# Moving the normalising operations out of block 0's groups, and a new order at the doors of a three-block gated layer

## What is computed

```python
# 4 batches, 8 heads, 576 positions, 64 wide
ret = (q @ k.T / 8) * Dmat            # Dmat: gamma ** (i - j) below the diagonal
x = (ret @ v)                         # as rows: 2304 tokens x 512
rms = np.sqrt(np.mean(x * x, axis=-1, keepdims=True) + 1e-06)
xn = x / rms * rms_g
g = xn @ w_gate                       # 512 -> 1536
val = xn @ w_val
x = silu(g) * val @ w_out             # 1536 -> 512, silu(g) = g * sigmoid(g)
...                                   # then the routed layer
```

## Time and profile before

| | us |
|---|---|
| median of 3 timed runs | 882.36 (881.67 to 883.47) |
| the profiled execution | 893.08 |
| its span | 891.1 |
| busy in the span: PE, DVE, POOL, ACT | 803.2, 519.7, 450.9, 425.7 |
| granted PE clock, mean | 0.964 |

### The profile page before, as it was taken

One profiled execution on the slowest core, in us unless ns is written; L12 is line 12 of the kernel. 1 busy time (PEld: TensorE's weight loads), 2 busy tenths in 40 slices (PEclk: granted clock), 3 DMA queues, 4 the chain that ended last, 5 costly groups with the idle time before them and its releaser, 6 DMA issues.

```text
span 891.1 us, 14837 instructions
## 1 busy us (share of the span) xinstructions
PE 803.2 (90%) x5053; PEld 706.5 (79%) x5053; DVE 519.7 (58%) x798; ACT 425.7 (48%) x815; POOL 450.9 (51%) x384
## 2 busy tenths in 40 slices
PE   7997688877899999789999999972999999999995
PEld 6886578776679999667999978842888888888884
DVE  3577678998535888653688632351455454554553
ACT  3564464444445555354655423521355454455453
POOL 3568976667754888664688523156112112222221
PEclk9998899999999999799999999987999999999998
DMA  9982012113121223212124012311545545556553
GB/s 317 318 285 86 24 49 70 48 48 95 48 60 36 72 88 125 76 55 60 29 76 143 28 47 67 123 37 32 172 144 163 185 155 169 177 160 173 161 169 103
DMA packets 48362, 99.65 MB, mean 112 GB/s; under 512 B 7490, under 2 KB 8644, under 8 KB 48295
## 3 DMA queue, kind: packets, MB, share of 16 engines
q1 hardware_dynamic: 42934, 87.40, 31.1%
q0 software_dynamic: 4944, 10.96, 4.2%
q10 hardware_dynamic: 432, 0.63, 0.2%
HBM read 89.50 MB, written 10.40 MB: 112 GB/s over the span
## 4 chain that ended last, share of the span: by engine, by line
PE 70%; POOL 10%; DVE 9%; issue 5%; ACT 3%; another core or an unknown queue 2%; DMA 1%; SPq 0%; POOLq 0%; ACTq 0%; DVEq 0%
PE banks L1392 7%; PE banks L1394 6%; PE banks L1393 6%; PE banks L1446 5%; PE banks L1579 5%; PE banks L1580 5%; PE banks L1448 5%; PE banks L1447 5%; PE banks L1581 5%; PE banks L1379 4%; PE banks L1380 4%; PE banks L1381 4%; POOL AL L493 3%; POOL AL L487 2%
## 5 line engine op out<-in xcount | busy, mean ns | idle before, releaser
L1392 PE MATMUL banks<-BH,AH 128*128 128x384 f32 x504 | 175.4, 348 | 29.7 <-DVE g L779 13.3
L1393 PE MATMUL banks<-BL,AH 128*128 128x384 f32 x504 | 171.2, 340 | 0.0
L1394 PE MATMUL banks<-BH,AL 128*128 128x384 f32 x504 | 171.1, 339 | 0.0
L1392 PEld LDWEIGHTS banks<-BH,AH 128*128 128x128 f32 x504 | 96.0, 191 | 41.5 <-DVE g L779 16.5
L809 DVE TENSOR_TENSOR hidL<-hid,hidH 128x384 fp32r<-128x384 f32 x72 | 55.8, 780 | 91.9 <-ACT hidH L1086 91.9
L493 POOL TENSOR_TENSOR AL<-s_ab,AH 128x1024 fp32r<-128x1024 f32 x36 | 94.7, 2631 | 12.5 <-ACT AH L1064 12.3
L1446 PE MATMUL banks<-dH,hidH 128*128 128x512 f32 x216 | 87.4, 405 | 12.9 <-DVE hidL L809 12.9
L1394 PEld LDWEIGHTS banks<-BH,AL 128*128 128x128 f32 x504 | 96.4, 191 | 0.0
L1393 PEld LDWEIGHTS banks<-BL,AH 128*128 128x128 f32 x504 | 96.2, 191 | 0.0
L505 POOL TENSOR_TENSOR dL<-wraw,dH 128x512 fp32r<-128x512 f32 x36 | 49.0, 1362 | 85.6 <-ACT dH L1079 85.6
L1579 PE MATMUL banks<-wH,h2H 128*112 128x512 f32 x192 | 77.7, 405 | 14.4 <-DVE h2L L963 14.4
(11 more groups left out here) (179 smaller groups left out, 1723.2 us busy)
## 6 DMA issues: line engine op xcount, KB each, us to landing
wraw<-w_moe SPq DMA_DIRECT2D x168, 256.0 KB, 2.7
wraw<-w_moe SPq DMA_DIRECT2D x36, 512.0 KB, 3.6
vr<-v_rows SPq DMA_DIRECT2D x15, 320.0 KB, 4.6
qt<-q_t SPq DMA_DIRECT2D x16, 288.0 KB, 4.6
y_rows<-y_sb SPq DMA_DIRECT2D x6, 768.0 KB, 6.0
kt<-k_t SPq DMA_DIRECT2D x15, 288.0 KB, 4.3
kr<-k_rows SPq DMA_DIRECT2D x16, 256.0 KB, 3.2
mask<-c_mask SPq DMA_DIRECT2D x4, 160.0 KB, 5.5
```

Of the source, the lines that this page charges most:

```text
L1392: mm(to, wh, bh, start=first and k == 0, stop=False, skip_group_check=True)
L1393: mm(to, wh, bl, start=False, stop=False, skip_group_check=True)
L1394: i = mm(to, wl, bh, start=False, stop=k == 1, skip_group_check=True)
```

## The change

Five things are done.

- **Normalising.** In block 0's first phase one task a group is left, behind the first hidden product (`IN_UP`: three root steps of batch 2, then eight multiplications). The rest (`IN_DOWN`, eleven tasks) stands in the second phase, one a step. Batches 2 and 3 get their own tiles (`late`).
- **Split of the first inner rows.** For groups 0 and 1 DVE makes all four inner rows (`sums_four`), and it makes the low parts of T3 and NT4 of block 0 (`low_first`).
- **Attention's end.** The sum of batch 2 is made one unit later, and the lists behind the units are rearranged on ACT, DVE and POOL. Batch 3's mean square comes before the sigmoid table is loaded. PE's order at the entry of a block is m2, m1, m5.
- **Doors of the second phase.** The two halves of step 0 stand inside the last group, one between m6 and m7, one between m7 and m4; high and low parts of its hidden tile are made in the groups 10 and 11.
- **Second phase.** The sums and splits of the next block's token parts are spread over other steps and stand between or behind the two halves; the second half's results are taken out in the next block's first groups; the first two loads of outer weights are queued in group 2.

```diff
-            return SCORES + 1 if b == BATCH - 1 else out_bank((b + 1) * PAIRS) + 1
+            return (out_bank(PAIRS) + 1, out_bank(2 * PAIRS) + 1, out_bank(3 * PAIRS + 1) + 1, SCORES + 1)[b]
...
+        DOWN_B = {0: B21, 1: B11, 2: B22, 3: T1, 5: T2, 6: T3, 7: NT4}
...
             for blk in range(BLOCKS):
                 n0 = blk * F1
                 for f in range(F1):
+                    if f >= F1 - 2:
+                        low_down(n0 + f - F1 + 2)
                     sums_a(n0 + f + 2)
                     low_a(n0 + f + 2)
                     low_S(n0 + f + 2)
                     low_b22(n0 + f + 2)
-                    if f >= F1 - 2:
-                        low_down(n0 + f - F1 + 2)
...
+            def sums_four(n):
+
+                sums_two(n)
+                r = wraw[:, n % 2, :]
+                dve.wait_ge(s_Sd, 4 * n + 1)
+                V.tensor_tensor(s_ab[:, 1, :], s_ab[:, 0, :], r[:, 0:HK], ALU.subtract).then_inc(s_Sd, 1)
+                dve.wait_ge(s_Sd, 4 * n + 3)
+                V.tensor_tensor(s_ab[:, 3, :], r[:, HK:2 * HK], s_ab[:, 1, :], ALU.subtract).then_inc(s_Sd, 1)
+
+            def low_first(b):
+
+                dve.wait_ge(s_BH, b + 1)
+                V.tensor_tensor(BL[:, b], t3[:] if b == T3 else x_part(0, b), BH[:, b].bitcast(F32),
+                                ALU.subtract).then_inc(s_BLd, 1)
...
                 if u == 9:
-                    sums_two(0)
+                    sums_four(0)
                 if u == 13:
-                    sums_two(1)
                     sums_b(0, T3)
                     sums_b(0, T1)
                 if u == 14:
-                    root(2, HALVE, TIMES)
-                    normalise(2, 0)
+                    sums_b(0, T2)
                 if u == 15:
-                    sums_b(0, T2)
                     sums_b(0, NT4)
-                    root(2, FIX)
+                    sums_four(1)
...
+            low_first(T3)
+            low_first(NT4)
...
                 V.tensor_tensor(hv[:, 1:2, :], g1[:], sig[:, 1:2, :], ALU.mult).then_inc(s_hv1, 1)
+                run(between)
...
                 V.tensor_tensor(hid[:, f:f + 1, HALF:BLOCK], hv[:, 1:2, :], v1[:], ALU.mult).then_inc(s_h1, 1)
-                for task in more[0:1]:
-                    task()
+                run(then)
                 dve.wait_ge(s_m4, n + 1)
                 dve.wait_ge(s_hv0, n + 1)
                 V.tensor_tensor(hid[:, f:f + 1, 0:HALF], hv[:, 0:1, :], x, ALU.mult).then_inc(s_h0, 1)
-                for task in more[1:]:
-                    task()
+                run(last)
...
-            LATER = ([norm_task(2, k) for k in range(1, KD)] + [norm_task(3, k) for k in range(KD)] + [root_task(3, i) for i in range(3)]
-                     + [norm_task(4, k) for k in range(KD)] + [norm_task(5, k) for k in range(KD)])
+            IN_UP = [root_task(2, i) for i in range(3)] + [norm_task(q, k) for q in (2, 3) for k in range(KD)]
+            IN_DOWN = [root_task(3, i) for i in range(3)] + [norm_task(q, k) for q in (4, 5) for k in range(KD)]
+            DOWN_T = {0: T3, 1: T1, 4: T2, 6: NT4}
             for blk in range(BLOCKS):
                 n0 = blk * F1
                 for f in range(F1):
-                    hidden(n0 + f, LATER[2 * f:2 * f + 2] if blk == 0 else ())
-                low_hidden(2 * n0)
-                low_hidden(2 * n0 + 1)
+                    hidden(n0 + f, [low_task(2 * n0 + 1)] if f == F1 - 1 else (), IN_UP[f:f + 1] if blk == 0 else (),
+                           [low_task(2 * n0)] if f == F1 - 2 else ())
                 for f in range(F1):
...
                     if f < F1 - 1:
                         low_hidden(2 * (n0 + f + 1))
+                    if blk + 1 < BLOCKS and f in DOWN_T:
+                        sums_b(blk + 1, DOWN_T[f])
+                    if f < F1 - 1:
                         low_hidden(2 * (n0 + f + 1) + 1)
+                    if blk == 0:
+                        run(IN_DOWN[f:f + 1])
...
+                if blk > 0 and f < TPH:
+                    take_y(blk - 1, 1, f)
+                if f == F1 - 3:
+                    high_down(n - f)
+                if f == F1 - 2:
+                    high_hidden(2 * (n - f))
+                    high_hidden(2 * (n - f) + 1)
+                    high_down(n - f + 1)
...
-                if u > 0 and u % PAIRS == 0:
+                if u in (PAIRS, 2 * PAIRS, 3 * PAIRS + 1):
                     norm(u // PAIRS - 1)
...
             for blk in range(BLOCKS):
                 n0 = blk * F1
                 m2(n0)
-                m5(n0)
                 if blk == 0:
                     norm_last()
+                m1(n0)
+                m5(n0)
                 for n in range(n0, n0 + F1):
-                    m1(n)
+                    last = n == n0 + F1 - 1
+                    if n > n0:
+                        m1(n)
                     m3(n)
                     m6(n)
-                    if n + 1 < n0 + F1:
+                    if last:
+                        down1(n0, 0)
+                    else:
                         m2(n + 1)
                     m7(n)
-                    if n + 1 < n0 + F1:
+                    if last:
+                        down1(n0, 1)
+                    else:
                         m5(n + 1)
                     m4(n)
-                for n in range(n0, n0 + F1):
-                    down1(n)
+                for n in range(n0 + 1, n0 + F1):
+                    down1(n, 0)
+                    down1(n, 1)
```

More of the change, by code:

```diff
@@ L169, in build @@
         hid = sb_in(h_stack, "hid", [P, F1, BLOCK])
+        late = sb_in(h_stack, "late", [P, 4, SEQ])
         h_stack.close()
@@ L305, in build, with statistics, inverse @@
         DOWN = ((0, 6, 2), (3, 4, 5))
+        def statistics(b):
+            return (late[:, 3, :], late[:, 2, :]) if b == BATCH - 1 else (ms[:, b % 2, :], r0[:, b % 2, :])
+        def inverse(b):
+            return rinv[:, b, :] if b < 2 else late[:, b - 2, :]
         def x_part(blk, b):
@@ L395, in _ @@
                     weights1_up(n0 + f + 4)
+                    if blk == 0 and f == 2:
+                        for p in range(2):
+                            sp.dma_start(wraw[:, p, UPC:W1COLS], plane(w_moe1, p)[:, UPC:W1COLS]).then_inc(s_wd[p], 16)
                     if f >= F1 - 2:
@@ L679, in root @@
                     if part_no == HALVE:
-                        wait(dve, s_xnf, KD * {0: 0, 1: 0, 2: 1, 3: 3}[b])
                         dve.wait_ge(s_ms, b + 1)
@@ L770, in _, with run, hidden @@
                 lag(u)
-            def hidden(n, more=()):
+            low_first(T3)
+            low_first(NT4)
+            def run(tasks):
+                for task in tasks:
+                    task()
+            def hidden(n, between=(), then=(), last=()):
                 x, f = banks[:, X[n % 2]:X[n % 2] + 1, 0:HALF], n % F1
@@ L1191, in _ @@
                     up_step(n0 + f)
-                high_hidden(2 * n0)
-                high_hidden(2 * n0 + 1)
                 for f in range(F1):
                     down_step(n0 + f, blk)
-                evacuate_y(blk, 0)
-                if blk + 1 < BLOCKS:
-                    evacuate_y(blk, 1)
+                for j in range(TPH):
+                    take_y(blk, 0, j)
             act.wait_ge(s_down, BLOCKS * 2 * F1)
```

164 lines of the change are left out of this document (85 added, 79 removed).

## The result

| | us |
|---|---|
| change, median of 10 runs | 889.21 (887.03 to 891.75) |
| before, beside it, median of 10 runs | 883.66 (881.60 to 886.45) |
| ratio | 1.0056, 95% interval 1.0038 to 1.0074 |
| the profiled execution after | 890.16, span 888.3, clock 0.982 |

A forecast was written before the change was run, and what follows sets the result against it. It looked for PE's waits at the attention's end, block 0's groups, doors and second phases. Gains of 11.6, 2.4, 5.2, 8.5 and 2.0 made 29.7 off 893.08; 863.4 times 0.988 gave 853 us, range 837 to 868.

The forecast's parts named there:

- Part 4: Second phases: fewer stalls and one step less behind the door; 5.2, 8.5 and 2.0 us gained in blocks 0, 1, 2.
- rival (c): Block 0's second phase: each normalising operation holds up hidL, 34 us lost, 884 to 889 in all; chance 0.03.
- eleven steps of 4.08: Second phases: steps left behind the door, eleven instead of twelve, 4.08 us each, counted as 44.9 us.
- Part 3: Doors between phases: first down step's halves fill the last group; 10.1 us from its first addition to the second step.
- m3 wait: Entry of a block: m3 waits for the copy of m5, 0.5 us in block 0, 0.6 in block 1.
- Part 1: Way into the expert layer: work moved from POOL to DVE brings the first addition to 90.5; 11.6 us gained.
- Rival (b): Way in bound by DVE behind POOL: gives back 5 to 9 us, about 860; chance 0.26 with (d).
- (d): Doors not opened: blocks 1 and 2 give 4 instead of 10.5 us, 859; chance 0.26 with Rival (b).
- Part 2: Block 0's groups: one normalising operation a group, groups of about 9.5 us; only 2.4 us gained.
- Rival (a): Block 0's groups fall into block 1's fast pattern: another 10 to 20 us, about 838; chance 0.13.
- The scale: Whole kernel: the profiled forecast of 863.4 us times 0.988, timed median over profiled execution, gives 853.0.
- no half clock in block 1's second phase: Sign expected in the new trace, block 1's second phase, where the clock was 0.93 over the old window.

The follow-up runs named there:

- e1: The change with both hidden halves put ahead of the high part of the outer weights again in the second phases; 883.60 us, ratio 0.9892.
- e2: The kernel before with the high part of the outer weights moved between the two hidden halves; 911.72 us, ratio 1.0215.
- f6: f1 with the doors shut: both halves of step 0 and their high and low parts behind the last group; 868.25 us, ratio 0.9717.
- f1: The change with the three edits of e1, e3 and e7 together; 853.24 us, ratio 0.9678.
- f5: f1 with PE taking m5 ahead of m1 at the entry of blocks 1 and 2; 861.76 us, ratio 0.9641.
- e3: e1 with group 0's second two inner rows back on POOL; 882.09 us, ratio 0.9879.
- e4: e1 with the normalising operation in block 0's groups one column wide from group 3 on; 882.36 us in one run.
- e7: e1 with block 0's normalising operation right behind the first two inner rows, ahead of g's second half; 857.22 us, ratio 0.9730.
- e5: The change itself once more, unaltered, in another set; 887.50 us, ratio 1.0049.
- e8: e1 with the low part of the first hidden product made in the last group, not at the end of group 10; 873.13 us, ratio 0.9888.
- f4: f2 with the edit of e8 added; 856.91 us, ratio 0.9736.
- f2: f1 with PE taking m5 ahead of m1 in blocks 1 and 2 and ACT copying m5 earlier in block 0; 854.67 us, ratio 0.9692.

## Why the prediction was wrong

It missed by 36 us at the routed layer (29.7 forecast, 6.2 lost). In its own steps:

**Part 4, the second phases: the step that failed.** "The high part of B now follows the second hidH, so POOL starts it behind hidL, which frees most hidL" looked at what comes behind the second hidH and not at what now comes ahead of it. The diff shows `high_down` between the two halves, but the sum kept "eleven steps of 4.08". Shown by e1 and e2: 14.8 us. With the order restored the last groups and second phases gain 2.9, 5.4 and 1.2 us (e1), 9.5 instead of 15.7: gains of the forecast kind are there, mis-sized by 6.2 us more, of which the door below is one part. I named rival (c), slower through the second phases, but for the normalising operations in block 0 and with 0.03; what came was ACT's order, in all three blocks. That (c)'s sum also ends at 889 is chance.

**Part 3, the doors.** Right in kind, and f6 puts the whole at 5.6 us. But from the last group's first addition to the second step I counted 10.1 us with one wait of 2.3; it took 11.6, 11.5 and 9.9, in f1 11.5 with two waits, 1.25 ahead of the half inside the group and 1.82 ahead of the second step. What I booked at nothing was the price in the first phases: the low part at the end of group 10 and POOL's `low_down` at the head of its lists, 2.3 us in block 1. f6 holds both the gain and most of this price, so 1.9 us a block is what is left of them.

**The entry of a block.** Of the m3 wait I counted 0.6 for block 1, 0.8 for block 2 with the clock, and 0.5 "inside this" for block 0. f5 shows 1.8 and 1.7 us for blocks 1 and 2; in block 0 PE waits 2.83.

**Part 1, the way in.** 11.6 forecast, 5.3 measured, inside its bounds of 2 to 14. From the attention's end to the first addition it took 8.25 us, 8.5 forecast; what was wrong is the attention's end, put at 82 and measured at 88.6. I had looked at the wait that goes and not at what the two extra inner rows of group 0 put in front of the scores on DVE; they took four times their bare time or more, and the scores behind them held PE for 3.25 us (e3, 3.4 us back; its attention ends at 84.5, so 2.5 us are mis-sized otherwise). That the later stretch came out at 8.25 is in part luck: I took two of its eight instructions as caught, and of the eight between 86.05 and 96.84 five took at least twice their bare time, but the first started 2.5 us before the attention's end. Rival (b), which I gave 0.26 with (d), had the size (5 to 9 us) and the mechanism, at another place. The Trainium skill (SBUF — State Buffer, Who interferes with whom) says that a DVE instruction with two SBUF inputs contends with a GpSimd instruction that reads SBUF. It follows that work moved from POOL to DVE stays on the shared pair; this pointed the right way, and I weighed the rows of one group above it.

**Part 2, block 0's groups.** Forecast 9.5 us a group and measured 9.45; 2.4 against 0.7 is the first group (10.4 us) and the low part at the end of group 10 (10.5). The reading of place and size was right and e4 sharpens it: even one column pays for the wait. One reading was loose: L796 does not end with L493 but 0.42 us behind it (200.18 and 199.76 in the earlier trace rows), so that a caught product costs the rest of POOL's instruction and most of its own time. Rival (a), the fast pattern, had 0.13 and "nothing ahead of L796 changes" against it; e7 shows that it lies one placement away and is worth 16.4 us over the eleven groups.

**The scale.** I multiplied by 0.988 to go from the profiled execution to the median. Of the difference, 10.7 us, some 9 go with one wait in the routed layer (last section), not with a stretching of the rest; the subtraction should have been made on 882.36 directly. Here it makes 0.3 us.

That f1 has 853.24 us, the number forecast, is a coincidence: it is made of other terms.

## What to carry to other kernels

Where two instructions of an in-order engine are released by the same event, the one that the bottleneck waits for should stand first; read this for every pair whose order a diff changes, also where both look cheap. Where DVE and POOL take turns, don't ask how long an added operation is but which POOL instruction it will stand behind and which one it will hold up: the same operation in three places made groups of 9.45, 8.98 and 7.69 us. Busy time of DVE is no bound as long as its instructions take longer than bare; compare each with its shortest duration first.

## What the runs showed of the hardware that was not expected

**One wait in the routed layer comes and goes.** In the traces of before, e1 to e4, f5 and f6 ACT waits once at the start of the routed layer for something that the trace calls remote; timeline of ACT in the kernel before:

```profile
620.72 0.45 ACT L1265 ACTIVATE h2H<-banks 128x336 fp32r<-128x336 f32 x1 [16.86 <-remote]
```

It was 15.1 to 16.9 us long, PE stood for 12 to 15 us of it, and after, e5 to e8 and f1 to f4 have no such wait. It goes with the set of experiments, not with the kernel: in the two sets whose traces have it before took 892.3 and 893.1 us, in the others 883.5 and 881.9. From the routed layer's start to the end of the span it is 286 to 288 us with the wait and 275 to 280 without. Nor does it go with the chip: the set of e5 to e8 and that of f5 and f6 ran on the same one. The first profiled execution of before, 893.08, has it too, beside timed runs of 882.36. What it is I did not find out.

**A wait of the same length at full clock and at half.** At block 2's door PE waits 1.98 us in f1 and 1.98 in f2, followed by the same matmuls. Windows of f1 and of f2 right behind it (clock is the third last number):

```profile
493.00:497.00 4.00, 4.00 (x19) 3.28 (x19) 0.72 (x2) 1.24 (x3) 0.00 (x0) 1.00 0.08 29
```

```profile
493.00:497.00 4.00, 4.00 (x12) 3.15 (x12) 0.56 (x1) 0.52 (x1) 0.00 (x0) 0.61 0.00 0
```

f2 falls to half clock there (0.61 over the window), f1 stays at 1.00, and its second phase is 1.6 us shorter. Ten traces have this wait, 1.98 or 1.99 us long; nine of them fall and only f1 doesn't. Block 1 shows the same with one and the same kernel: behind a wait of 1.82 us in after and 1.81 in e5, which is after once more, windows of after and of e5:

```profile
369.00:379.00 10.00, 7.63 (x32) 5.69 (x32) 7.52 (x6) 3.36 (x6) 6.30 (x4) 1.00 0.37 119
```

```profile
368.50:378.50 10.00, 8.94 (x27) 6.41 (x26) 5.84 (x5) 2.83 (x5) 4.45 (x3) 0.66 0.33 105
```

Block 1's last group and second phase took 68.9 us there and 70.7 here. So "no half clock in block 1's second phase" came true in one trace of two. A sum over an edit that leaves such a wait has to carry that spread.
